# One layer change in a routed expert kernel: gathers, weight pieces, a rounding and two blocks in another order

## The chip, the core and the metric

The kernel runs on one core of a Trainium2 chip. The metric is the device time of one execution in microseconds. The core's engines are named as in the profile: PE (TensorE, matmuls), DVE (VectorE), ACT (ScalarE), POOL (GpSimd) and SP (SyncE, which here only issues DMAs). Each runs its own instructions in order and waits for the others by semaphores.

## What is computed

Three layers in a row, all in float32: a gated recurrent attention ("mixer", not touched by the change), then a mixture of experts in which each of 8 experts takes 384 of the 3072 tokens, then a two-layer ELU network over all tokens.

```python
# mixture of experts: the (token, expert) pairs in falling order of logit, each expert full at cap
cap = N // E                      # 3072 // 8 = 384
for idx in np.argsort(-(x @ w_gate).flatten()):
    tok, e = idx // E, idx % E
    if assigned[tok] < 0 and counts[e] < cap:
        assigned[tok] = e; counts[e] += 1
for e in range(E):
    h = np.maximum(x[assigned == e] @ w1[e], 0.0)      # 320 -> 1024
    out[assigned == e] = h @ w2[e]                     # 1024 -> 320
# second network, every token
h = x @ w_in                                           # 320 -> 2048
g = np.where(h > 0.0, h, np.exp(np.minimum(h, 0.0)) - 1.0)
y = g @ w_out                                          # 2048 -> 320
```

## The kernel before

The mixer fills the first 200 us or so and stores x by rows. Then the experts are done one after the other, each with its 384 tokens through both networks before the next begins. `experts_in_turn` writes the body out for experts 0 and 1, runs experts 2 to 5 in a hardware loop, two at a time, and writes out 6 and 7. The order of the work on each engine is written by hand, in one block per engine; nothing is planned by a tool.

**Two roundings.** Each float32 operand is kept as a high part, rounded by ACT, and a low part, what is left (by DVE or POOL), and a product is made of three: high by high, high by low, low by high.

**One expert on PE.** Eight hidden blocks: `up` (eight matmuls of 384 columns, a "block" of the first layer) and `down` two blocks behind. Then the change of layer, and sixteen blocks f of the second network: `up2(f)` (eight matmuls, made by `rows_product`), and `down2(f - 3)` (nine matmuls of 320 columns), three blocks behind (LAG). Three PSUM banks go round between the `up` blocks, so `up2(f)` waits for the ELU of block f - 3 (`g_ok`). In blocks 12 to 14 (TURN) PE transposes the next expert's rows (`columns`); behind the last blocks it starts the next expert's first two `up`.

**Change of layer.** `between_layers`: ACT copies a folded part (L1476), rounds two thirds of the result (L1479), then the last third (L1481, L1482); DVE adds the folded part (L1351) and makes the low parts (L1354, L1356). `up2(0)` waits part by part; its last matmul (L1622) needs L1356.

**ELU of a block.** ACT: ReLU of the negative (L1489), tanh (L1492), exp (L1497). DVE: L1362 and L1365, which gives g. ACT rounds g of the block before (`elu_hi`, L1504). POOL makes its low part (`elu_lo`, L1109). Then `down2` may start (first matmul L1684).

**Weights.** The next expert's weights come in eight pieces (0 to 3 of w1, 4 to 7 of w2), by way of two staging buffers. SP may fetch piece m when the low part of piece m - 2 is done. ACT rounds it (`piece`, L845 and L846, or L847 for w2), POOL makes the low part (`expert_rest`, L855 and L858, or L863 and L864). In the loop this happens in the even blocks 0 to 14, one piece each. For expert 0 it is done ahead of the loop: ACT rounds pieces 0 to 3, then the gathered columns, then pieces 4 to 7 with `hidden(0, 0)` behind piece 6 and `hidden(0, 1)` behind piece 7.

**Routing.** While expert k runs, DVE and PE choose expert k + 2's tokens in six rounds. Each has a comparison on DVE (the first in three slices, L756, behind the ELU of blocks 1 to 3; later ones L1194), a count on PE (L1559, or L1565 and L1573 where it is folded), a test on DVE (L1207, L1209, giving feas), the thresholds on PE (L1579), and a move of the base on DVE (L1216, L1218). During the eight hidden blocks the choice is finished: counts, ties, and the "spots" (L1320), from which PE lists the tokens (L1594) and DVE makes `idx` (L1331). POOL then gathers their rows in three indirect DMAs (L1088). The keys of the following routing (`choose_start`, `choose_keys`) stand on DVE ahead of `between_layers`. For expert 0 and 1 the rounds run ahead of the loop; `hidden(0, 0)` stands on DVE between rounds 3 and 4 of expert 1's, `hidden(0, 1)` between rounds 5 and 6.

## Time and profile before

| what | value |
|---|---|
| median of 3 runs | 884.07 us (883.91 to 884.22) |
| the profiled execution | 882.67 us, its span 880.9 us |
| PE busy | 780.1 us, 89% of the span |
| PE weight loads | 715.2 us, 81% |
| DVE busy | 547.3 us, 62% |
| ACT busy | 460.7 us, 52% |
| POOL busy | 402.7 us, 46% |
| granted TensorE clock, mean | 0.960 of full |

The rest of the 882.67 us lies around the span. The expert stage runs from about 230 us to the end. A matmul's row in the profile lasts longer than the distance to the next one, since they overlap: distances are read from start to start. A square bracket at the end of a row gives the idle time of the engine before it and what ended it.

### The profile page before, as it was taken

The page shows a single profiled execution, that of the slowest core. Times are in us where ns is not written, and L with a number is a line of the kernel's source. Part 1 is how long each engine was busy: PE and PEld are TensorE (multiplying, and loading weights), DVE is VectorE, ACT ScalarE, POOL GpSimd, SP SyncE. Part 2 cuts the span into 40 slices and gives each one's busy share as a digit, 9 for nine tenths or more (in the row PEclk, how much of TensorE's full clock was granted, in tenths as well). Part 3 has the DMA queues.
Part 4 walks back from the last instruction along what each step waited for, and adds up shares of the span by engine and source line. Part 5 has one row for each costly group of instructions (what it writes and reads, how often), then busy time and mean ns, then how long its engine had stood idle before and what let it go on. Part 6 is the DMA issues. An engine that isn't in the chain of part 4 may idle for free.

```text
span 880.9 us, 18310 instructions
## 1 busy us (share of the span) xinstructions
PE 780.1 (89%) x5822; PEld 715.2 (81%) x5822; DVE 547.3 (62%) x1586; ACT 460.7 (52%) x981; POOL 402.7 (46%) x469
## 2 busy tenths in 40 slices
PE   1999999993158999999999999999999999999994
PEld 1888888882148899889979988997898899899894
DVE  7576768686865774666577467647647664543441
ACT  1544444431231675387277538726753872784573
POOL 6544444443460464176246417624650752474133
PEclk9999999996558999999999999999999999999998
DMA  3766666633331221121122012121201212220000
GB/s 66 146 135 136 135 135 134 136 74 94 102 106 43 58 56 36 54 84 32 65 60 56 34 53 85 31 69 52 58 31 54 78 45 65 57 69 23 1 1 22
DMA packets 138516, 61.04 MB, mean 69 GB/s; under 512 B 104704, under 2 KB 136704, under 8 KB 138432
## 3 DMA queue, kind: packets, MB, share of 16 engines
q1 hardware_dynamic: 136128, 52.13, 24.5%
q0 software_dynamic: 2304, 7.87, 2.8%
q8 instruction: 43, 0.70, 0.3%
q14 instruction: 41, 0.34, 0.1%
HBM read 51.72 MB, written 8.26 MB: 68 GB/s over the span
## 4 chain that ended last, share of the span: by engine, by line
PE 45%; DVE 11%; ACT 7%; issue 5%; POOL 4%; DMA 2%; SPq 2%; ACTq 0%; DVEq 0%; POOLq 0%
PE bank L1684 6%; PE bank L1686 5%; PE bank L1685 5%; PE bank L1614 5%; PE bank L1618 5%; PE bank L1615 5%; DVE unit L1320 3%; PE bank L1622 3%; PE bank L1620 2%; DMA stage<-in_moe_w_dram 2%; PE bank L1660 2%; PE bank L1658 2%; PE bank L1659 2%; ACT unit L1492 1%; POOL xg L1088 1%
## 5 line engine op out<-in xcount | busy, mean ns | idle before, releaser
L1109 POOL TENSOR_TENSOR gl_lo<-unit,gl_hi 128x384 fp32r<-128x384 f32 x128 | 131.2, 1025 | 142.9 <-ACT gl_hi L1504 142.6
L1684 PE MATMUL bank<-Wo_hi,gl_hi 128*128 128x320 f32 x384 | 125.9, 328 | 8.2 <-POOL gl_lo L1109 8.2
L1686 PE MATMUL bank<-Wo_hi,gl_lo 128*128 128x320 f32 x384 | 118.8, 309 | 0.0
L1685 PE MATMUL bank<-Wo_lo,gl_hi 128*128 128x320 f32 x384 | 118.7, 309 | 0.0
L1362 DVE SCALAR_TENSOR_TENSOR unit<-bank,unit 128x384 f32<-128x384 f32 x104 | 57.8, 556 | 94.2 <-ACT bank L1497 86.3
L1472 ACT ACTIVATE hid_hi<-bank 128x384 fp32r<-128x384 f32 x64 | 31.4, 491 | 135.8 <-PE bank L1622 132.1
L1088 POOL DMA_INDIRECT xg<-x_rows,idx x24 | 23.3, 972 | 159.5 <-DVE idx L1331 82.9
L1614 PE MATMUL bank<-x_hi,Wi_hi 128*128 128x384 f32 x256 | 92.7, 362 | 1.9 <-DVE unit L1365 0.9
L1489 ACT ACTIVATE unit<-bank 128x384 f32<-128x384 f32 x128 | 62.0, 484 | 49.6 <-PE bank L1622 49.5
L1615 PE MATMUL bank<-x_hi,Wi_lo 128*128 128x384 f32 x256 | 86.1, 336 | 0.0
L1684 PEld LDWEIGHTS bank<-Wo_hi,gl_hi 128*128 128x128 f32 x384 | 72.6, 189 | 12.9 <-POOL gl_lo L1109 12.9
L1365 DVE TENSOR_TENSOR unit<-unit,bank 128x384 f32<-128x384 f32 x128 | 70.9, 554 | 4.4
L1685 PEld LDWEIGHTS bank<-Wo_lo,gl_hi 128*128 128x128 f32 x384 | 72.4, 188 | 0.0
L1686 PEld LDWEIGHTS bank<-Wo_hi,gl_lo 128*128 128x128 f32 x384 | 72.1, 188 | 0.0
L1492 ACT ACTIVATE unit<-unit 128x384 f32<-128x384 f32 x128 | 67.3, 525 | 4.4
L1618 PE MATMUL bank<-x_lo,Wi_hi 128*128 128x384 f32 x256 | 67.9, 343 | 1.4 <-DVE x_lo L1354 1.0
L1345 DVE SCALAR_TENSOR_TENSOR hid_lo<-bank,hid_hi 128x384 fp32r<-128x384 f32 x64 | 35.5, 554 | 53.4 <-ACT hid_hi L1472 52.8
L1504 ACT CAST gl_hi<-unit 128x384 fp32r<-128x384 f32 x128 | 63.7, 498 | 6.3 <-DVE unit L1365 6.3
L316 POOL TENSOR_SCALAR_AFFINE_SELECT W<-W 128x512 f32<-128x512 f32 x48 | 36.1, 775 | 57.7 <-ACT W L505 57.7
L444 DVE TENSOR_TENSOR PW<-bank,W 128x512 f32<-128x512 f32 x48 | 30.9, 686 | 40.5 <-PE bank L566 40.4
L1614 PEld LDWEIGHTS bank<-x_hi,Wi_hi 128*128 128x128 f32 x256 | 48.2, 188 | 8.4 <-DVE unit L1365 3.6
L1497 ACT ACTIVATE bank<-unit 128x384 f32<-128x384 f32 x104 | 51.6, 496 | 3.3
(256 smaller groups left out, 2081.8 us busy)
## 6 DMA issues: line engine op xcount, KB each, us to landing
stage<-in_moe_w_dram SPq DMA_DIRECT2D x32, 320.0 KB, 3.0
stage<-in_moe_w_dram SPq DMA_DIRECT2D x32, 256.0 KB, 2.6
stage<-in_moe_w_dram SPq DMA_DIRECT2D x96, 64.0 KB, 2.4
q_in<-in_q_dram SPq DMA_DIRECT2D x24, 160.0 KB, 2.6
k_in<-in_k_dram SPq DMA_DIRECT2D x24, 160.0 KB, 3.1
o_in<-in_o_gate_dram SPq DMA_DIRECT2D x24, 160.0 KB, 3.3
v_in<-in_v_dram SPq DMA_DIRECT2D x24, 160.0 KB, 3.4
x_rows<-xt SPq DMA_DIRECT2D x24, 160.0 KB, 1.8
```

The source lines that it names most:

```text
L1109: nc.gpsimd.tensor_tensor(gl_lo[:, b, :], ex[:, b, :], gl_hi[:, b, :].bitcast(F32), ALU.subtract).then_inc(gl_ok, 1)
L1362: nc.vector.scalar_tensor_tensor(out=ex[:, b, :], in0=exp_at(f), scalar=1.0, in1=th[:, f % 2, :], op0=ALU.add, op1=ALU.mult).then_inc(em_o ...
L1365: nc.vector.tensor_tensor(ex[:, b, :], ex[:, b, :], ring[(NF + f) % 3][:, 0:CAP], ALU.max).then_inc(g_ok, 1)
L1489: nc.scalar.activation(ex[:, b, :], ring[(NF + f) % 3][:, 0:CAP], ACT.Relu, scale=-1.0).then_inc(neg_ok, 1)
L1492: nc.scalar.activation(th[:, f % 2, :], ex[:, b, :], ACT.Tanh, scale=-0.5).then_inc(th_ok, 1)
L1504: nc.scalar.copy(gl_hi[:, b, :], ex[:, b, :]).then_inc(gl_hi_ok, 1)
L1614: nc.tensor.matmul(to, w_hi[:, c, cols], x_hi[m][:, c, :], start=(c == 0), stop=False)
L1615: nc.tensor.matmul(to, w_lo[:, c, cols], x_hi[m][:, c, :], start=False, stop=False)
L1618: nc.tensor.matmul(to, w_hi[:, c, cols], x_lo[m][:, c, :], start=False, stop=False)
L1684: nc.tensor.matmul(acc[j][:, 0:DM], gl_hi[:, f % RG, t_], Wo_hi[:, f, :], start=(f == 0), stop=False)
L1685: nc.tensor.matmul(acc[j][:, 0:DM], gl_hi[:, f % RG, t_], Wo_lo[:, f, :], start=False, stop=False)
L1686: ins = nc.tensor.matmul(acc[j][:, 0:DM], gl_lo[:, f % RG, t_], Wo_hi[:, f, :], start=False, stop=(f == NF2 - 1))
```

## The change

- The gathers of the next expert are issued on POOL after the low parts of blocks 0, 1 and 2, one each, and no longer all ahead of block 0. For expert 0 they come ahead of all its weight pieces on POOL, and ACT's columns come ahead of pieces 2 and 3.
- Pieces 0 to 6 move from the even blocks 0 to 12 to the odd blocks 3 to 15. Piece 7 (`LATE`) goes into the next expert: behind hidden block 2 on ACT, and first on POOL.
- ACT's ELU is split into `elu_tanh` and `elu_exp`; in block 1 the rounding of block 0's result stands between the two.
- `up2(0)` and `up2(1)` become `up2_first_two`: four products of block 0, four of block 1, then the low and last ones of block 0, then those of block 1.
- On DVE `choose_keys` moves behind `between_layers` and `choose_tokens`, ahead of the first ELU; the test of a folded round moves from ahead of the even block to right behind the ELU of the odd one.
- Expert 0's spots read the slots from SBUF in fp16 as all others do; the float32 copy in PSUM (`slots_p`) is gone.

The diff, without the lines that only drop the parameter `waits` of `rows_product`:

```diff
@@ -700,7 +700,6 @@
         self.cmp_w = sb("cmp", [P, G * first_n + 2], BF16)
         self.ramp1_p = bank[7][:, 176:176 + first_n]
         self.ramps_p = bank[7][:, 304:304 + (len(STEPS) - 1) * 33].rearrange("p (q n) -> p q n", n=33)
-        self.slots_p = bank[6][:, 384:512]
         self.early = sem("r_early")
         self.const, self.zeroed, self.done = sem("r_const"), sem("r_zero"), sem("r_init")
         self.first_ok = sem("r_first")
@@ -788,7 +787,6 @@
             nc.vector.tensor_scalar(self.ramps_p[:, q, 0:n], self.ramp_i[:, low:low + n],
                                     step * (1.0 if q + 1 < HIGH else UNIT), None, ALU.mult)
         nc.vector.tensor_copy(self.ramp1_p, self.ramp1[:])
-        nc.vector.tensor_copy(self.slots_p, self.slots_i[:])
         nc.vector.tensor_copy(self.slots[:], self.slots_i[:])
         nc.vector.tensor_copy(self.rows2[:], self.rows_i[:])
         nc.vector.tensor_copy(self.marks[:], self.marks_i[:])
@@ -1005,6 +1003,9 @@
     block = ctx.enter_context(nc.Block())
+    def first_expert(k):
+        return isinstance(k, int) and k == 0
+
     def passed(eng, s, value):
         if not isinstance(value, int) or value > 0:
@@ -1042,6 +1043,11 @@
     LAG = 3
     TURN = NF2 - NJ - 1
+
+    def piece_beside(f):
+        return (f - 3) // 2 if f > 2 and f % 2 else None
+
+    LATE = PER - 1
     def exp_at(f):
         return ex[:, f % RG, :] if TURN <= f < TURN + NJ else pEx
@@ -1080,13 +1086,13 @@
         for m in range(2):
             nc.gpsimd.memset(x_lo[m][W3:P, 2, :].bitcast(F32), 0.0).then_inc(x_pads, 1)
-        def gather(k, s):
-            pool.wait_ge(idx_ok, k + 1)
-            passed(pool, x_pe_part, k * NJ)
-            pool.sem_inc(pool_turn)
-            for j in range(NJ):
-                nc.gpsimd.indirect_dma_start(out=xg[:, j, :], out_offset=None, in_=x_rows[:, :],
-                                             in_offset=bass.IndirectOffsetOnAxis(ap=idx[s][:, j:j + 1], axis=0)).then_inc(x_in[j], 16)
+        def gather(k, s, j):
+            if j == 0:
+                pool.wait_ge(idx_ok, k + 1)
+                passed(pool, x_pe_part, k * NJ)
+                pool.sem_inc(pool_turn)
+            nc.gpsimd.indirect_dma_start(out=xg[:, j, :], out_offset=None, in_=x_rows[:, :],
+                                         in_offset=bass.IndirectOffsetOnAxis(ap=idx[s][:, j:j + 1], axis=0)).then_inc(x_in[j], 16)
         def scatter(k, s):
             for j in range(NJ):
@@ -1111,20 +1117,20 @@
         pool.wait_ge(x_pads, 2)
         for i in range(PI):
             rest(False, w_out_piece(i), i, i % 2, OUT_SPLIT)
+        for j in range(NJ):
+            gather(0, 0, j)
         for i in range(PER):
             expert_rest(0, i)
-            if i == 1:
-                gather(0, 0)
         def body(k, s, n, after):
-            if after:
-                pool.wait_ge(up_pe, k * UP + NF)
-                pool.wait_ge(mid_pe, k * 3 + 3)
-                gather(k + 1, 1 - s)
+            if not first_expert(k):
+                expert_rest(k, LATE)
             for f in range(NF2):
                 elu_lo(k, f)
-                if f % 2 == 0 and after:
-                    expert_rest(k + 1, f // 2)
+                if f < NJ and after:
+                    gather(k + 1, 1 - s, f)
+                if piece_beside(f) is not None and after:
+                    expert_rest(k + 1, piece_beside(f))
             scatter(k, s)
         experts_in_turn(pool, body)
@@ -1154,9 +1160,6 @@
             return (B - 1 + k) * KEY_STEPS
         SLICES = 3
-
-        def first_expert(k):
-            return isinstance(k, int) and k == 0
         def all_or_last(k):
             return (slice(G - G // B, G), G // B) if first_expert(k) else (slice(0, G), G)
@@ -1317,8 +1320,7 @@
             n = G // SPOTS
             for g in range(part * n, (part + 1) * n):
-                ins = nc.vector.tensor_scalar(spot[:, g, :], tables.slots_p if first_expert(k) else slots[:], row[:, g:g + 1],
-                                              None, ALU.is_equal)
+                ins = nc.vector.tensor_scalar(spot[:, g, :], slots[:], row[:, g:g + 1], None, ALU.is_equal)
             ins.then_inc(spot_ok, 1)
         def choose_tokens(k, s, n):
@@ -1420,24 +1422,25 @@
                 hidden(k, u)
             if after == 2:
                 choose_start(c + 1)
-                choose_keys(c + 1)
             between_layers(k)
             if after:
                 choose_tokens(c, 1 - s, n + s)
             for f in range(NF2):
                 q, odd = f // 2 - 1, f % 2
                 if after == 2:
-                    if q >= 1 and odd:
+                    if f == 0:
+                        choose_keys(c + 1)
+                    elif q >= 1 and odd:
                         if q in FOLDED:
                             round_parts(c + 1, q)
                         else:
                             round_test(c + 1, q)
                     elif q >= 2:
-                        if q - 1 in FOLDED:
-                            round_test(c + 1, q - 1)
                         round_move(c + 1, q - 1)
                         round_compare(c + 1, q)
                 elu(k, f)
+                if after == 2 and odd and q in FOLDED:
+                    round_test(c + 1, q)
                 if 1 <= f <= SLICES and after == 2:
                     compare_first(c + 1, f - 1)
                 if TURN <= f < TURN + NJ and after:
@@ -1481,7 +1484,7 @@
             nc.scalar.copy(x_hi[1][W3:2 * W3, 2, :], whole3)
             nc.scalar.copy(x_hi[1][0:W3, 2, :], whole3).then_inc(mid_hi_ok, 1)
-        def elu(k, f, after):
+        def elu_tanh(k, f):
             u, b = k * NF2 + f + 1, f % RG
             act.wait_ge(up_pe, k * UP + NF + f + 1)
@@ -1490,6 +1493,10 @@
             act.wait_ge(neg_ok, u)
             passed(act, em_ok, u - 2)
             nc.scalar.activation(th[:, f % 2, :], ex[:, b, :], ACT.Tanh, scale=-0.5).then_inc(th_ok, 1)
+
+        def elu_exp(k, f, after):
+
+            u, b = k * NF2 + f + 1, f % RG
             act.wait_ge(th_ok, u)
             passed(act, em_ok, u - 1)
             if f == TURN + NJ and after:
@@ -1510,10 +1517,12 @@
         for i in range(PI):
             piece(False, i, w_out_arrival(i), OUT_SPLIT)
-        for i in range(PE1):
+        for i in range(2):
             piece(True, i, expert_arrival(0, i), W1_SPLIT)
         for j in range(NJ):
             columns(0, j)
+        for i in range(2, PE1):
+            piece(True, i, expert_arrival(0, i), W1_SPLIT)
         for i in range(PE1):
             piece(False, i, expert_arrival(0, PE1 + i), W2_SPLIT)
             if i > 1:
@@ -1522,14 +1531,18 @@
         def body(k, s, n, after):
             for f in range(2, NF):
                 hidden(k, f)
+                if f == 2 and not first_expert(k):
+                    piece(False, LATE % PE1, expert_arrival(k, LATE), W2_SPLIT)
             between_layers(k)
             for f in range(NF2):
-                elu(k, f, after)
-                if f > 0:
+                elu_tanh(k, f)
+                if f == 1:
+                    elu_hi(k, 0)
+                elu_exp(k, f, after)
+                if f > 1:
                     elu_hi(k, f - 1)
-                if f % 2 == 0 and after:
-
-                    i = f // 2
+                i = piece_beside(f)
+                if i is not None and after:
                     piece(i < PE1, i % PE1, expert_arrival(k + 1, i), W1_SPLIT if i < PE1 else W2_SPLIT)
                 if TURN <= f < TURN + NJ and after:
                     columns(k + 1, f - TURN)
...
@@ -1665,17 +1674,35 @@
         def up2(k, f):
             r = NF + f
-            if f < 3:
-                pe.wait_ge(hid_ok, k * NF + NF - 2 + f)
+            if f == 2:
+                pe.wait_ge(hid_ok, k * NF + NF)
             else:
                 pe.wait_ge(g_ok, k * NF2 + f - 2)
-
-            def waits(c, lo):
-
+            rows_product(ring[r % 3][:, 0:CAP], Wi_hi, Wi_lo, f, 1).then_inc(up_pe, 1)
+
+        def up2_first_two(k):
+
+            to = [ring[(NF + f) % 3][:, 0:CAP] for f in range(2)]
+            for f in range(2):
+                cols = slice(f * P, (f + 1) * P)
+                pe.wait_ge(hid_ok, k * NF + NF - 2 + f)
+                for c in range(2):
+                    if f == 0:
+                        pe.wait_ge(mid_hi_ok, k * 3 + c + 1)
+                    nc.tensor.matmul(to[f], Wi_hi[:, c, cols], x_hi[1][:, c, :], start=(c == 0), stop=False)
+                    nc.tensor.matmul(to[f], Wi_lo[:, c, cols], x_hi[1][:, c, :], start=False, stop=False)
+            for f in range(2):
+                cols = slice(f * P, (f + 1) * P)
+                for c in range(2):
+                    if f == 0:
+                        pe.wait_ge(mid_ok, k * 3 + c + 1)
+                    nc.tensor.matmul(to[f], Wi_hi[:, c, cols], x_lo[1][:, c, :], start=False, stop=False)
                 if f == 0:
-                    pe.wait_ge(mid_ok if lo else mid_hi_ok, k * 3 + c + 1)
-
-            rows_product(ring[r % 3][:, 0:CAP], Wi_hi, Wi_lo, f, 1, waits).then_inc(up_pe, 1)
+                    pe.wait_ge(mid_hi_ok, k * 3 + 3)
+                nc.tensor.matmul(to[f], Wi_hi[:, 2, cols], x_hi[1][:, 2, :], start=False, stop=False)
+                if f == 0:
+                    pe.wait_ge(mid_ok, k * 3 + 3)
+                nc.tensor.matmul(to[f], Wi_hi[:, 2, cols], x_lo[1][:, 2, :], start=False, stop=True).then_inc(up_pe, 1)
         def down2(k, f):
             pe.wait_ge(gl_ok, k * NF2 + f + 1)
@@ -1728,7 +1755,9 @@
                 list_tokens(c)
             down(k, NF - 1)
             for f in range(NF2 + LAG):
-                if f < NF2:
+                if f == 0:
+                    up2_first_two(k)
+                elif 1 < f < NF2:
                     up2(k, f)
                 q = f // 2 - 1
                 routing = after == 2 and f < NF2 and q >= 1
```

## Rows read from the trace of the kernel before

**Rows 1.** Busy time by stretches, one middle expert: us, busy (x instructions), PEclk, DMA.

```profile
377.00:454.00 77.00, 74.39 (x533) 68.46 (x532) 49.65 (x154) 46.47 (x102) 36.20 (x38) 1.00 0.18 55
```

**Rows 2.** Timeline of PE at the third expert's layer change: start us, us, engine line.

```profile
443.83 0.34 PE L1660 MATMUL bank<-hid_lo,W_split 128*128 128x384 f32 x1
...
446.83 0.45 PE L1622 MATMUL bank<-x_lo,Wi_hi 128*128 128x384 f32 x1
...
450.30 0.44 PE L1614 MATMUL bank<-x_hi,Wi_hi 128*128 128x384 f32 x1 [0.24 <-DVE unit L1365]
...
453.03 0.41 PE L1684 MATMUL bank<-Wo_hi,gl_hi 128*128 128x320 f32 x1 [1.07 <-POOL gl_lo L1109]
```

**Rows 3.** Timeline, same stretch: the first block's ELU on ACT, DVE and POOL.

```profile
447.40 0.49 ACT L1489 ACTIVATE unit<-bank 128x384 f32<-128x384 f32 x1 [1.21 <-PE bank L1622]
...
448.99 0.60 ACT L845 CAST W_hi<-stage 128x512 fp32r<-128x512 f32 x1
...
449.69 0.56 DVE L1365 TENSOR_TENSOR unit<-unit,bank 128x384 f32<-128x384 f32 x1
...
451.40 0.50 ACT L1504 CAST gl_hi<-unit 128x384 fp32r<-128x384 f32 x1
...
451.98 0.99 POOL L1109 TENSOR_TENSOR gl_lo<-unit,gl_hi 128x384 fp32r<-128x384 f32 x1 [0.20 <-ACT gl_hi L1504]
```

**Rows 4.** Timeline: hand-over to the second layer, third expert, then seventh (PE).

```profile
443.13 0.48 ACT L1476 COPY unit<-bank 64x384 f32<-64x384 f32 x1 [3.29 <-PE bank L1643]
...
444.59 0.54 DVE L1351 TENSOR_TENSOR unit<-bank,unit 64x384 f32<-64x384 f32 x1
...
753.21 0.34 PE L1660 MATMUL bank<-hid_lo,W_split 128*128 128x384 f32 x1
...
755.76 0.44 PE L1622 MATMUL bank<-x_lo,Wi_hi 128*128 128x384 f32 x1
```

**Rows 5.** Timeline, third expert: two waits of PE, and DVE before the second.

```profile
468.65 0.18 PE L1579 MATMUL bank<-feas,first 128*128 128x1 bf16 x1 [0.24 <-DVE feas L1209]
...
486.55 0.55 DVE L1365 TENSOR_TENSOR unit<-unit,bank 128x384 f32<-128x384 f32 x1
...
488.14 0.18 PE L1579 MATMUL bank<-feas,first 128*128 128x1 bf16 x1 [0.49 <-DVE feas L1209]
```

**Rows 6.** Timeline, third expert: last slice of the first comparison, then its count.

```profile
457.29 1.21 DVE L756 SCALAR_TENSOR_TENSOR cmp<-hi,bank 128x1016 bf16<-128x1016 f32 x1
...
458.78 0.76 PE L1559 MATMUL bank<-pick,cmp 128*128 128x8 bf16 x24
```

**Rows 7.** The page, costliest groups: the gathers. Busy us, mean ns, idle before, releaser.

```profile
L1088 POOL DMA_INDIRECT xg<-x_rows,idx x24 | 23.3, 972 | 159.5 <-DVE idx L1331 82.9
```

**Rows 8.** Timeline of the start of the expert stage, DVE, ACT, POOL and PE.

```profile
234.05 6.29 DVE L1320 TENSOR_SCALAR unit<-bank,row 128x128 f16<-128x128 f32 x24
...
283.70 2.04 DVE L1320 TENSOR_SCALAR unit<-slots,row 128x128 f16<-128x128 f16 x12
...
235.68 0.62 ACT L845 CAST W_hi<-stage 128x512 fp32r<-128x512 f32 x1 [7.90 <-DMA stage<-in_moe_w_dram]
...
236.79 1.26 POOL L855 TENSOR_TENSOR W_lo<-stage,W_hi 128x512 fp32r<-128x512 f32 x1 [7.39 <-ACT W_hi L846]
...
242.77 1.28 POOL L1088 DMA_INDIRECT xg<-x_rows,idx  x1 [1.45 <-DVE idx L1331]
...
243.04 0.62 ACT L845 CAST W_hi<-stage 128x512 fp32r<-128x512 f32 x1 [3.74 <-DMA stage<-in_moe_w_dram]
...
246.57 1.28 POOL L855 TENSOR_TENSOR W_lo<-stage,W_hi 128x512 fp32r<-128x512 f32 x1
...
257.95 0.48 ACT L1472 ACTIVATE hid_hi<-bank 128x384 fp32r<-128x384 f32 x1
...
258.59 0.55 DVE L1345 SCALAR_TENSOR_TENSOR hid_lo<-bank,hid_hi 128x384 fp32r<-128x384 f32 x1
...
268.37 0.67 PE L1614 MATMUL bank<-x_hi,W_hi 128*128 128x384 f32 x1
```

More of the change, by code:

```diff
@@ L1607, in columns, with rows_product @@
             ins.then_inc(x_pe_part, 1)
-        def rows_product(to, w_hi, w_lo, f, m, waits):
+        def rows_product(to, w_hi, w_lo, f, m):
             cols = slice(f * P, (f + 1) * P)
             for c in range(2):
-                waits(c, 0)
                 nc.tensor.matmul(to, w_hi[:, c, cols], x_hi[m][:, c, :], start=(c == 0), stop=False)
@@ L1616, in rows_product @@
             for c in range(2):
-                waits(c, 1)
                 nc.tensor.matmul(to, w_hi[:, c, cols], x_lo[m][:, c, :], start=False, stop=False)
-            waits(2, 0)
             nc.tensor.matmul(to, w_hi[:, 2, cols], x_hi[m][:, 2, :], start=False, stop=False)
-            waits(2, 1)
             return nc.tensor.matmul(to, w_hi[:, 2, cols], x_lo[m][:, 2, :], start=False, stop=True)
```

2 lines of the change are left out of this document (1 added, 1 removed).

## Prediction

> **What bounds the kernel now.** I read the busy times by stretches first [rows 1], then PE's timeline for its holes. In a middle expert PE is busy 74.4 of 77.0 us at full granted clock, so time can be won there only where PE stands still, and in the start of the expert stage, where it hardly works. In a middle expert there are three kinds of hole.
>
> *The change of layer* [rows 2]. From the last product of the first layer (443.83) to the first output product of the second (453.03) are 9.20 us, in which PE has four blocks of eight matmuls to do, about 1.4 us each. Some 3.6 us are idle: about 1.0 before the end of block 0 (446.83), 0.4 before block 3 (450.30, waiting for DVE), 1.2 before 453.03 (waiting for POOL's low part). The last hole is ScalarE's order [rows 3]: the first ReLU starts at 447.40, DVE is through with block 0 at 450.25 (449.69 + 0.56), but gl_hi begins only at 451.40, because ACT had put a weight piece (448.99) and all three steps of block 1 ahead of it. POOL's gl_lo follows at 451.98 and PE at 453.03.
>
> *The hand-over* [rows 4]. ACT has the folded part at 443.61 (443.13 + 0.48); DVE takes it up at 444.59, behind the keys of the next routing. In the seventh expert, which makes no keys, block 0 ends 2.55 us after the last product (753.21, 755.76); in the first six it is 2.83 to 3.03 (third: 3.00).
>
> *The routing's tests* [rows 5]. PE waits 0.24 us for feas before block 8's output product and 0.49 us in block 14. The second is there in all six experts that route, 0.49 to 0.52 us.
>
> **The change part by part**, gains negative, against the profiled execution (span 880.9, 882.67 in all; the median of the three runs is 884.07, 1.4 more, and I move that by the same sum).
>
> *Keys behind the hand-over.* The eight key instructions (about 1.0 us together, by which DVE is late at 444.59 [rows 4]) move to before the first ELU, where DVE waits for ACT's exp of block 0, which ends when the piece starts (448.99) [rows 3]; that idle time hides them, and uncovered they would cost their 1.0 us per expert. Then block 0 should end 2.55 to 2.6 us after the last product, as in expert seven: -0.35 on the mean, times 6 = **-2.0**.
>
> *First two blocks interleaved.* Four products of block 1 go into the hole in front of block 0's low parts. Block 0 ends when its last x_lo comes, as before, and the ELU starts from that. PE gets 0.7 us ahead, and then waits longer before block 3, which needs DVE's result of block 0. I take it at **0** by itself; its bounds are -0.3 (the hole of 0.4 before block 3) and +0.1.
>
> *Order of ACT: ReLU and tanh of block 1, then gl_hi of block 0, then exp of block 1; weight piece in block 3 instead of 0.* Exp of block 0 ends about 449.0, where the piece starts [rows 3]. ReLU and tanh of block 1, 0.5 us each like the first ReLU, end at 450.1, before DVE is through (450.25). So gl_hi runs 450.3 to 450.8, gl_lo 450.9 to 451.9, and PE starts at 451.95 instead of 453.03: -1.1. PE is not itself later: block 3 is through at 450.30 + 1.5 = 451.8 [rows 2]. Seven experts have a piece there. The eighth has none, and gains 0.2 at most, which I leave out. What is late next is the first comparison [rows 6]: its third slice ends at 458.50 and PE counts at 458.78. The slices follow ELU 1, 2 and 3 on DVE (1.1 us each beside 1.1 us of ELU), so they move up only with exp 1, 0.3 us, and by the 0.4 that the piece took out of block 2 before: the count starts some 0.8 us earlier, not 1.1. Of the other 0.3, most comes back by block 8, where the test waits 0.24 now, since ACT has done two pieces by then and not four. So -1.1 x 7 = -7.7, with a low end of -0.8 x 7 = -5.6: I take **-7.4**.
>
> *Gathers behind the first low parts.* POOL issues the three gathers, 0.97 us each on the mean [rows 7] and 0.3 between them, now after gl_lo 0, 1 and 2, and no longer ahead of them. Queued behind each is the next gl_lo. gl_lo 0 ends at 451.9, gather 0 at 453.2, gl_lo 1 can be done at 454.4, and PE wants it after output product 0 and block 4, at 454.8: hidden by 0.4 us. The two after have over 2 us. **0**. The rows of x are wanted only in block 12.
>
> *Tests right after the odd blocks.* For q 2 to 4 DVE's order stays what it was (nothing lies between). For q = 5 it does not: the test now comes before the columns of block 13, so it can start at 487.1, when the ELU of block 13 is done [rows 5]. It takes 0.35 us, so feas is there at 487.5, when PE ends block 14 (488.14 less the wait of 0.49 and the refill of 0.1): the wait of 0.49 and the refill of 0.1 go: -0.6 x 6 = **-3.6**. Bounds -0.3 and -0.6 each.
>
> *Weight pieces later.* Pieces 0 to 6 in blocks 3 to 15, the eighth behind the next expert's hidden 2. A hidden block gives ACT one rounding of 0.5 us [rows 8] in some 2.8 us of PE (two times eight matmuls), so one piece more finds room; POOL's part stands behind the scatter, and PE wants it only with the last two of eight hidden blocks, some 17 us into the layer. **0**; without that cover 0.7 each.
>
> *The start* [rows 8] is where the change costs. The slots from SBUF in fp16 make the spots shorter: 24 took 6.29 us, and 12 of the other form took 2.04, so 24 take 4.0: idx comes 2.3 us earlier, and the first gather starts at 240.45 (was 242.77). But POOL now issues expert 0's gathers ahead of all its weight pieces, waiting for idx. Low part 0 began at 236.79; now it begins when three gathers are issued, at 240.45 + 3.80 (242.77 to 246.57) = 244.25, which is 7.5 us later. SP fetches piece 2 into its buffer only after that: from low part 0 to ACT's piece 2 were 6.25 us (236.79 to 243.04), and 1.1 more to POOL (235.68 to 236.79). So low part 2 begins at 251.6, where it was 246.57: **5.0 later**. From it a chain of two more fetches (pieces 4 and 6) leads to ACT's hidden 0, which stands behind piece 6: 11.4 us (257.95). That gives 263.0. DVE needs it (258.59 before, with no time to spare) between rounds 3 and 4 of expert 1's routing, and behind that wait stand rounds 4 to 6, whose end lets PE start block 2 (268.37). All of it moves by **+4.9**; rounds 1 to 3 finish 2.3 us earlier and wait. Bounds +4.0 and +6.0, from the spread of a fetch. PE is at the lower of its clock's two levels (1.2 and 2.4 GHz) here: that first matmul takes 0.67 us against 0.44 in row 450.30 [rows 2]. Eight of them at half the rate take about 2.8 us where 1.4 is usual, and if the rise comes one block later or earlier it is 1.4 more or less; I leave it at 0 and widen the range.
>
> By the Trainium skill, page "TensorE: Matmul & The Clock Gate", section "Part 1: The HAM clock gate", the clock follows how busy the array has been of late, in a window that runs freely; by that rule the longer stillness can't lower a clock that is low already, and the moment of the rise may shift. The 0.67 us agrees that it is low before and after; the sum is the same by rule and by row.
>
> Sum: -2.0 - 7.4 - 3.6 + 4.9 = **-8.1**; I keep 0.3 back for blocks 10 and 12, where the test is within 0.1 us of PE: -7.8. 882.67 - 7.8 = 874.9 for the profiled execution, **876.3** for the median.
>
> **The rivals.**
>
> *A start without cost.* If hidden 0 did not wait for the late pieces, 4.9 us stay in: 871.4. Against it speaks that 257.95 and 258.59 leave no slack now. 10%.
>
> *The first comparison takes the gain back.* DVE or ACT becomes the bound in blocks 3 to 8, and the 1.1 us of the routing experts are gone at the first count. Left are 2.0 + 3.6 + 1.1 (the seventh) - 4.9 = -1.8: 882.3. For it: PE's count follows the last slice by 0.3 us already [rows 6]. Against it: exp 1 comes earlier too. 15%, half of it inside 0.2%.
>
> *The gathers hold the low parts up: slower.* Each gather stands between two low parts. If it holds POOL for g us longer than its 0.97, beside DVE's ELU and comparison, gl_lo 3 is late by 3g - 2.5 in all seven experts (its slack is 2.5 us). The gain is gone at g = 1.2, and with g = 1.6 (a gather of 2.5 us) it is 7 x 2.3 = 16 us: 892. Against it: the mean of all 24 is 0.97 us [rows 7], and DVE works beside most of them now. For it: the very first one [rows 8] took 1.28. 8%.
>
> By the skill's page "SBUF — State Buffer", section "Who interferes with whom", writing a gather's descriptors is shut out while VectorE runs a two-port instruction, and that would be this rival; it also says that an instruction with a PSUM operand does not do it, which is what stands beside the gathers here, and no row of before shows a gather so held.
>
> The change as I read it, 876.3: 67%.
>
> **How the numbers follow.** A measurement of this kernel can tell 0.2%, 1.8 us: 882.3 to 885.8 is "the same". Faster: 67% + 10% + half of 15% = 84%, less 2% for what I haven't seen: 0.82. Same: 0.09. Slower: 0.09. The range goes from the start without cost (871.5) to the lost comparison (882.0). It leaves out the slower case and the tips of the other two.
>
> **What would show it.** Right: gl_hi of block 0 directly behind tanh of block 1, PE's first output product 4.9 to 5.1 us after block 0's last matmul (it was 6.0 to 6.2); block 0's end 2.6 us after the last product; no wait of L1579 in block 14; hidden 0 of expert 0 at 263 and block 2 at 273. Wrong: a PE wait of 1 us before the first count of each expert, gathers over 2 us, a hidden 0 that stays at 258, or a new PE hole in blocks 3 to 8.

## The result and the profile after

| | before | after |
|---|---|---|
| median | 883.99 us (882.93 to 884.22, 4 runs) | 873.54 us (872.99 to 874.11, 4 runs) |
| profiled execution, its span | 882.67, 880.9 | 872.99, 871.2 |
| PE's first count of expert 0 | 208.71 | 207.43 |
| *start*: from there to the last product of expert 0's first layer | 81.56 | 87.93 |
| *behind*: from there to the end of the span | 590.63 | 575.84 |

The ratio is 0.9884, interval [0.9867, 0.9901]: 10.4 us faster. 876.3 was forecast, with 871.5 to 882.0 around it. The three lower rows divide the span, and all runs below are read by them. The mixer, which nothing here touches, ends at different times from profile to profile (first count between 207.43 and 211.73), so a difference of 1 or 2 us in one median may be its doing; *start* and *behind* are free of it. Of the 9.7 us between the spans, -1.3 is the mixer, +6.4 the start and -14.8 what lies behind. For the last two the forecast was +4.9 and -12.7.

Timeline of PE of the kernel after, the third expert's layer change and its test in block 14 (start us, us, line, [idle before <- what ended it]); it answers [rows 2, 5, 6]:

```profile
444.67 0.34 PE L1669 MATMUL bank<-hid_lo,W_split 128*128 128x384 f32 x1
...
447.25 0.42 PE L1705 MATMUL bank<-x_lo,Wi_hi 128*128 128x384 f32 x1
...
450.68 0.45 PE L1626 MATMUL bank<-x_hi,Wi_hi 128*128 128x384 f32 x1 [0.92 <-DVE unit L1367]
...
452.31 0.41 PE L1711 MATMUL bank<-Wo_hi,gl_hi 128*128 128x320 f32 x1
...
486.67 0.18 PE L1592 MATMUL bank<-feas,first 128*128 128x1 bf16 x1
```

From the last product to block 0's last matmul are 2.58 us (3.00 before), and 7.64 to the first output product (9.20). The wait for POOL's low part is gone from the row 452.31; the wait for DVE ahead of block 3 (row 450.68) has grown from 0.24 to 0.92, and it is now the largest hole of the change of layer. The row of the test in block 14 has no bracket: PE waits no more. ACT, DVE and POOL, same stretch, answering [rows 3]:

```profile
449.88 0.52 ACT L1495 ACTIVATE unit<-unit 128x384 f32<-128x384 f32 x1
450.66 0.51 ACT L1511 CAST gl_hi<-unit 128x384 fp32r<-128x384 f32 x1 [0.25 <-DVE unit L1367]
451.08 0.49 ACT L1504 ACTIVATE bank<-unit 128x384 f32<-128x384 f32 x1
...
450.07 0.56 DVE L1367 TENSOR_TENSOR unit<-unit,bank 128x384 f32<-128x384 f32 x1
...
451.25 1.01 POOL L1115 TENSOR_TENSOR gl_lo<-unit,gl_hi 128x384 fp32r<-128x384 f32 x1 [20.73 <-ACT gl_hi L1511]
452.41 0.98 POOL L1094 DMA_INDIRECT xg<-x_rows,idx  x1 [0.15 <-issue]
453.57 1.02 POOL L1115 TENSOR_TENSOR gl_lo<-unit,gl_hi 128x384 fp32r<-128x384 f32 x1 [0.17 <-ACT gl_hi L1511]
```

gl_hi runs as soon as DVE is through with block 0 and not 1.2 us later, gl_lo behind it, and the gather (0.98 us) fits between two low parts: the second low part waits for ACT (0.17), not for the gather. The start, answering [rows 8]:

```profile
232.60 3.99 DVE L1323 TENSOR_SCALAR unit<-slots,row 128x128 f16<-128x128 f16 x24
...
239.01 1.29 POOL L1094 DMA_INDIRECT xg<-x_rows,idx  x1 [11.06 <-DVE idx L1333]
...
242.81 1.28 POOL L853 TENSOR_TENSOR W_lo<-stage,W_hi 128x512 fp32r<-128x512 f32 x1
...
249.95 0.62 ACT L843 CAST W_hi<-stage 128x512 fp32r<-128x512 f32 x1 [3.36 <-DMA stage<-in_moe_w_dram]
...
251.05 1.26 POOL L853 TENSOR_TENSOR W_lo<-stage,W_hi 128x512 fp32r<-128x512 f32 x1 [4.38 <-ACT W_hi L844]
...
262.34 0.48 ACT L1475 ACTIVATE hid_hi<-bank 128x384 fp32r<-128x384 f32 x1
...
265.25 0.34 PE L1578 MATMUL bank<-pick,cmp 128*128 128x32 bf16 x6 [7.76 <-DVE cmp L1197]
...
272.53 0.67 PE L1626 MATMUL bank<-x_hi,W_hi 128*128 128x384 f32 x1
```

POOL stands idle for 11.06 us, issues the gathers, and only then makes the first low part. Hidden 0 comes last, and behind it the routing: PE waits 7.76 us in one hole.

### The profile page after: what moved, and what is told of

The parts are those of the page before. It is cut to its first block, busy times and chain, and to the rows that moved or that the text cites. A ratio compares the mean times of both kernels' runs of the same rounds, so it can differ in the third digit from the quotient of the medians.

```text
span 871.2 us, 18302 instructions
## 1 busy us (share of the span) xinstructions
PE 773.0 (89%) x5822; PEld 716.4 (82%) x5822; DVE 546.6 (63%) x1585; ACT 461.9 (53%) x981; POOL 403.7 (46%) x469
## 4 chain that ended last, share of the span: by engine, by line
PE 60%; DVE 9%; ACT 2%; issue 2%; POOL 1%; DMA 1%; SPq 0%; ACTq 0%; DVEq 0%; POOLq 0%
PE bank L1711 7%; PE bank L1626 7%; PE bank L1629 6%; PE bank L1627 6%; PE bank L1713 6%; PE bank L1712 6%; PE bank L1631 3%; PE bank L1630 3%; PE bank L1667 3%; PE bank L1669 3%; PE bank L1668 3%; DVE cmp L755 3%; DVE unit L1364 2%; PE bank L1652 1%; PE bank L1655 1%
## 5 line engine op out<-in xcount | busy, mean ns | idle before, releaser
L1364 DVE SCALAR_TENSOR_TENSOR unit<-bank,unit 128x384 f32<-128x384 f32 x104 | 57.8, 556 | 84.0 <-ACT bank L1504 84.0
L1626 PE MATMUL bank<-x_hi,Wi_hi 128*128 128x384 f32 x224 | 80.4, 359 | 6.7 <-DVE unit L1367 6.7
L1627 PE MATMUL bank<-x_hi,Wi_lo 128*128 128x384 f32 x224 | 75.2, 336 | 0.0
L316 POOL TENSOR_SCALAR_AFFINE_SELECT W<-W 128x512 f32<-128x512 f32 x48 | 36.1, 776 | 56.8 <-ACT W L505 56.8
L1629 PE MATMUL bank<-x_lo,Wi_hi 128*128 128x384 f32 x224 | 57.3, 337 | 0.0
L491 ACT COPY xT<-bank 128x384 f32<-128x384 f32 x24 | 11.5, 478 | 76.7 <-PE bank L610 76.7
L1626 PEld LDWEIGHTS bank<-x_hi,Wi_hi 128*128 128x128 f32 x224 | 42.2, 188 | 9.2 <-DVE unit L1367 9.2
```

The source lines that it names most:

```text
L1364: nc.vector.scalar_tensor_tensor(out=ex[:, b, :], in0=exp_at(f), scalar=1.0, in1=th[:, f % 2, :], op0=ALU.add, op1=ALU.mult).then_inc(em_o ...
L1626: nc.tensor.matmul(to, w_hi[:, c, cols], x_hi[m][:, c, :], start=(c == 0), stop=False)
L1627: nc.tensor.matmul(to, w_lo[:, c, cols], x_hi[m][:, c, :], start=False, stop=False)
L1629: nc.tensor.matmul(to, w_hi[:, c, cols], x_lo[m][:, c, :], start=False, stop=False)
```

## The experiments

All medians stand against runs of the kernel before on the same chip (883.67 to 884.57). *Start* and *behind* come from each profiled execution.

| kernel | median, us | ratio, 95% | start | behind |
|---|---|---|---|---|
| before | 883.99 | | 81.56 | 590.63 |
| after | 873.54 | 0.9884 [0.9867, 0.9901] | 87.93 | 575.84 |
| e1_hidden_early | 868.04 | 0.9820 [0.9803, 0.9837] | 80.44 | 576.04 |
| u3_gathers_first | 878.49 | 0.9945 [0.9925, 0.9966] | 86.87 | 580.26 |
| u1_hi_behind_exp | 872.99 | 0.9878 [0.9857, 0.9899] | 87.65 | 574.76 |
| u2_pieces_even | 893.21 | 1.0114 [1.0092, 1.0136] | 87.24 | 595.84 |
| u7_pieces_and_gathers | 883.56 | 0.9982 [0.9965, 0.9999] | 86.72 | 584.15 |
| u4_keys_before | 876.76 | 0.9929 [0.9906, 0.9953] | 86.88 | 577.82 |
| u5_tests_even | 882.02 | 0.9974 [0.9959, 0.9990] | 86.74 | 582.74 |
| u6_blocks_apart | 874.59 | 0.9899 [0.9875, 0.9923] | 85.61 | 575.78 |
| e2_gather_behind_two | 873.31 | 0.9881 [0.9855, 0.9906] | 86.81 | 576.13 |
| b1_early_and_hi_behind | 865.47 | 0.9793 [0.9772, 0.9813] | 79.21 | 574.86 |
| b2_early_hi_two | 866.85 | 0.9815 [0.9789, 0.9841] | 81.33 | 574.81 |
| b3_early_hi_slots_psum | 867.38 | 0.9815 [0.9790, 0.9840] | 81.39 | 574.52 |

The start as the change made it shows the scatter of such a reading: eight kernels have it (after, and the u kernels), from 85.61 to 87.93, 86.96 on the mean. The kernel after is the longest of them, and of the start before there is one reading. *Behind* scatters by about 0.3 (575.78 to 576.13 in four kernels that differ in nothing that matters there). The u kernels each undo one part of the change and keep the rest.

**The cost of the start.** e1 puts hidden 0 of expert 0 ahead of ACT's second four pieces; all else stays.

```diff
+        hidden(0, 0)
                 ...
-            if i > 1:
-                hidden(0, i - 2)
+            if i == 0:
+                hidden(0, 1)
```

> The changed kernel with one thing moved on ACT, ahead of the loop: hidden 0 of expert 0 stands behind weight piece 3 (no longer behind piece 6) and hidden 1 behind piece 4. Theory of the forecast (DVE's rounds 4 to 6 wait for hidden 0, which waits for the late weight pieces): the 7.8 us that PE stands still between rounds 3 and 4 go to about 0, the first block of expert 0 behind round 6 starts at 264.3 instead of 272.5, and the kernel takes 865.2 us (8.3 less than 873.5). Rival (the late pieces themselves are what PE needs): the wait reappears before the first products with w2 and the gain is under 4 us, 870 or more.

The start fell to 80.44, 6.5 below the mean of 86.96, and the hole of 7.76 us is gone: the row of that count (260.22) has no bracket.

```profile
256.49 0.47 ACT L1475 ACTIVATE hid_hi<-bank 128x384 fp32r<-128x384 f32 x1
...
260.22 0.39 PE L1579 MATMUL bank<-pick,cmp 128*128 128x32 bf16 x6
...
267.54 0.67 PE L1627 MATMUL bank<-x_hi,W_hi 128*128 128x384 f32 x1
```

The mechanism holds, but the size came out smaller: 868.04 where I had 865.2, a gain of 5.5 us by the medians and not 8.3. I had taken the hole from the kernel after; in the eight kernels with this start it is 6.5 to 7.9 us. So the start waits for hidden 0, and hidden 0 for the pieces ahead of it on ACT. What makes these late is a question of its own. e2 keeps hidden 0 behind piece 6 and puts POOL's gathers back behind the low parts of pieces 0 and 1:

```diff
-        for j in range(NJ):
-            gather(0, 0, j)
         for i in range(PER):
             expert_rest(0, i)
+            if i == 1:
+                for j in range(NJ):
+                    gather(0, 0, j)
```

> The changed kernel with one part undone, in the start alone: POOL issues expert 0's three gathers behind the low parts of weight pieces 0 and 1, as the kernel before did, and not ahead of all of them. Hidden 0 keeps its new place behind piece 6 on ACT. Measured from PE's first count of expert 0 to the last product of its first layer, the start takes 81.6 us before and 87.0 on the mean of the eight kernels with the new start. My theory (the chain gathers, low part 0, fetch of piece 2, low part 2, pieces 4 and 6, hidden 0): low part 0 goes back to about 236, hidden 0 of expert 0 to about 257, and the start to 80.9 to 81.9; the rest of the kernel stays 575.8; ratio 0.982. Rival (the cost lies in ACT's new order, columns ahead of pieces 2 and 3, or in POOL's three gathers wherever they stand): the start stays over 85 and the ratio at 0.988.

My theory failed here: 86.81, where I had 80.9 to 81.9. DVE, POOL and ACT of this kernel:

```profile
234.43 6.62 DVE L1324 TENSOR_SCALAR unit<-slots,row 128x128 f16<-128x128 f16 x24
...
243.47 1.28 POOL L1094 DMA_INDIRECT xg<-x_rows,idx  x1 [1.78 <-DVE idx L1334]
...
247.70 0.37 ACT L1465 CAST x_hi<-bank 128x256 fp32r<-128x256 f32 x1 [8.04 <-PE bank L1620]
...
250.96 0.62 ACT L843 CAST W_hi<-stage 128x512 fp32r<-128x512 f32 x1
...
262.95 0.48 ACT L1476 ACTIVATE hid_hi<-bank 128x384 fp32r<-128x384 f32 x1
```

The low parts of pieces 0 and 1 do come early again, and piece 2 is fetched in time: its row on ACT (250.96) has no wait for a DMA. But ACT now takes the gathered columns ahead of piece 2, stands 8.04 us idle for them, and comes to piece 2 at 250.96, 41.3 us behind the first count. It was 42.5 in the kernel after, where POOL made it late, and 34.3 before. The change has two reasons for a late hidden 0: POOL's gathers ahead of the low parts, and ACT's columns ahead of pieces 2 and 3. I had priced the first and not the second. In the kernel after ACT is through with the columns and ready for piece 2 at 246.59 (249.95 less its wait of 3.36), which is 39.2 us behind the first count: the columns alone make piece 2 4.8 us later than before, and POOL's late low part adds 3.4. In e2 the columns alone made it 7.0, because there the gathers too come 2.2 us later than in the kernel after (33.8 us behind the first count, not 31.6), for the reason that follows. No run has POOL's new order with ACT's old one, so that POOL's part by itself is argued from its wait of 3.36 us.

The row of the spots holds a second surprise: 6.62 us, not 3.99. b2 shows it again. Below is the spots' tile in b2, then the form with slots in PSUM in the kernel before (duration ns min/median/max, first and last start us):

```profile
L1324 DVE TENSOR_SCALAR unit<-slots,row x24: 242/249/1308, 232.5 to 237.9; 128x128 f16<-128x128 f16 x24
```

```profile
L1320 DVE TENSOR_SCALAR unit<-bank,row x24: 343/343/351, 234.1 to 240.0; 128x128 f16<-128x128 f32 x24
```

In b2 POOL makes low parts beside the spots, of two instructions each (1.26 and 0.72 us, from 235.30 and from 237.84). Twenty-one of the 24 spots take 0.24 to 0.25 us. The other three start within 0.03 us of an instruction of POOL and end within 0.06 us of its end: 1.31 us from 235.31, 0.76 from 236.53 and 1.28 from 237.87. In e2 it is again three spots (1.28, 0.76 and 1.32 us). So a spot that meets a low part of POOL is held for the length of that instruction. Before, the same low parts (from 236.79 and 239.38) ran beside the PSUM form, and none of the 24 took over 351 ns.

The Trainium skill's page "SBUF — State Buffer", section "Who interferes with whom", says that a `tensor_scalar` in a two-port mode and a GpSimd instruction exclude each other for the whole instruction. The trace agrees, with 1308 ns for one spot, though no row tells the mode.

So the slots in SBUF are worth 2.3 us only because the gathers stand ahead of the low parts and POOL is idle beside the spots; with both low parts beside them they cost 0.3 (6.61 against 6.29).

**Gathers and pieces in the loop.** u3 issues all three gathers ahead of the first low part, u2 puts the pieces back into the even blocks 0 to 14, u7 does both. u3:

```diff
+            if after:
                 ...
+                for j in range(NJ):
+                    gather(k + 1, 1 - s, j)
             for f in range(NF2):
                 elu_lo(k, f)
-                if f < NJ and after:
-                    gather(k + 1, 1 - s, f)
```

> The changed kernel with the three gathers of the loop put back ahead of low part 0, all else as changed. The forecast gave this move 0 us: 873.5. Rival (POOL was a second lock of nearly the same height: in the kernel before the gathers ended at 451.8 and gl_hi at 451.9, so freeing ACT alone frees nothing): the first output product comes 1.1 us later in seven experts, 7.50 to 7.65 us after the last product of layer one become 8.6 to 8.8, and the kernel takes 873.5 + 7 x 1.1 = 881 us, less what the first count's wait of 0.27 us takes up in six of them: 879.5 to 881.

u2 (in u7 with the lines of u3):

```diff
-        return (f - 3) // 2 if f > 2 and f % 2 else None
+        return None if f % 2 else f // 2
-            if not first_expert(k):
-                expert_rest(k, LATE)
                 ...
```

> The changed kernel with the weight pieces back in the even blocks 0 to 14, none in the next expert. Theory of the forecast: the piece in block 0 puts ReLU and tanh of block 1 and gl_hi of block 0 0.9 us later in seven experts; the test before block 8 is late again by some 0.3. 873.5 + 7 x 0.9 + 6 x 0.2 = 881. Rival (the gathers alone made the 1.1 us): 873.5 to 875.

> The changed kernel with both put back: weight pieces in the even blocks 0 to 14 and the three gathers ahead of low part 0. Each alone cost: the pieces 19.3 us, the gathers 3.4 us (expert stage, counted from PE's first count to the end, 663.8 us in the changed kernel and 672.2 before). Theory 1 (the two stand in for each other: a gather between low parts is bearable only where no weight piece stands there too, on POOL): the stage is near that of the kernel before, less the earlier keys and tests, plus the longer start: 671 to 673 us, 11 less than with the pieces alone. Theory 2 (the costs add up): 686 us. Theory 3 (the even blocks as such cost the 19 us, by ACT): 683 us.

Behind the start, u3 costs 4.4, u2 20.0 and u7 8.3. For u3 the rival's mechanism came true and not its price: the first output product comes at 8.59 us (8.6 to 8.8 expected), but the first count only 0.5 us later, and 4.4 are lost instead of 6 to 7.5. For u2 my 881 was wrong by 12 us (893.21); I had priced only ACT's queue. For u7 theory 1 holds: from the first count to the end are 670.9 us, where it had 671 to 673, and not 683 or 686. In u3 the third gather still holds POOL when gl_hi is ready; POOL and PE:

```profile
451.45 0.95 POOL L1094 DMA_INDIRECT xg<-x_rows,idx  x1 [0.30 <-issue]
452.42 1.00 POOL L1115 TENSOR_TENSOR gl_lo<-unit,gl_hi 128x384 fp32r<-128x384 f32 x1
...
453.48 0.41 PE L1714 MATMUL bank<-Wo_hi,gl_hi 128*128 128x320 f32 x1 [0.92 <-POOL gl_lo L1115]
```

Most of what ACT's order wins at the first output product would be lost again at POOL (8.59 for 7.64, 0.95 us). Before, the gathers stood there without harm, since gl_hi was itself late [rows 3]. In u2 POOL has a gather and a piece's low part between the first two gl_lo:

```profile
457.66 1.01 POOL L1115 TENSOR_TENSOR gl_lo<-unit,gl_hi 128x384 fp32r<-128x384 f32 x1 [23.05 <-ACT gl_hi L1509]
458.81 0.99 POOL L1094 DMA_INDIRECT xg<-x_rows,idx  x1
459.82 1.30 POOL L853 TENSOR_TENSOR W_lo<-stage,W_hi 128x512 fp32r<-128x512 f32 x1
461.08 0.74 POOL L856 TENSOR_TENSOR W_hi<-stage,W_hi 128x256 fp32r<-128x256 f32 x1
461.77 0.99 POOL L1115 TENSOR_TENSOR gl_lo<-unit,gl_hi 128x384 fp32r<-128x384 f32 x1
...
462.82 0.42 PE L1707 MATMUL bank<-Wo_hi,gl_hi 128*128 128x320 f32 x1 [1.12 <-POOL gl_lo L1115]
...
468.02 0.62 ACT L843 CAST W_hi<-stage 128x512 fp32r<-128x512 f32 x1 [3.16 <-DMA stage<-in_moe_w_dram]
```

The second gl_lo starts 4.1 us after the first (2.3 after the change), and PE waits. The low part of piece 0 ends 0.8 us later than in u7 (11.29 us after the last product for 10.48), and so is the fetch of piece 2 later: ACT stands 3.16 us for it in block 4, with the ELU queued behind. Over the seven experts this wait is 1.8 to 3.2 us, in u7 0.6 to 2.1. The third expert is 1.5 us behind the kernel after at its first count (15.11 for 13.61) and 3.1 at the test of block 8 (26.21 for 23.14), and loses no more behind that. How the 3.1 divide between PE's waits for gl_lo and ACT's for the fetch is not shown: the experts are 2.7 to 3.0 us longer whether ACT stands 1.8 us or 3.2.

u2 is slower than before by 1.1%, the only kernel here that is. Counted from u7, where neither move is made, the pieces' move alone (u3) wins 3.9 us, the gathers' move alone (u2) loses 11.7, and both together win 8.3. The two moves have to be priced as one.

**The other parts.** u1 puts the rounding of block 0 behind both steps of block 1:

```diff
-                if f == 1:
-                    elu_hi(k, 0)
-                if f > 1:
+                if f > 0:
```

> The changed kernel with gl_hi of block 0 back behind exp of block 1. Theory of the forecast: ACT is 0.3 us later with gl_hi in all eight experts, the first output product too; in the six experts that route exp 1 and with it the three slices of the first comparison come 0.5 us earlier, so the count's wait of 0.27 us pays for it. Net +0.1 us each there and +0.3 in the last two: +1 us, 874.5. Rival (the order within block 1 is what gained the 1.1 us, not the piece and the gathers): +7 us, 880.

*Behind* fell by 1.1, where I had expected 1 more (the medians, 872.99 and 873.54, are too close to tell; b1, b2 and b3, which have the same order, show 574.5 to 574.9 too). In the third expert the first output product is 0.2 later (7.85 instead of 7.64), but the first count is 0.24 earlier (13.37 instead of 13.61), and the time from expert to expert goes with the count: 0.26 less in the experts that route, 0.2 more in the last two. ACT's exp of block 1, ahead of the rounding, starts DVE's ELU 1 sooner, and the first comparison's slices stand behind that. u4 moves the keys back to where they were:

```diff
+                choose_keys(c + 1)
                 ...
-                    if f == 0:
-                        choose_keys(c + 1)
                 ...
```

> The changed kernel with the keys back ahead of the hand-over on DVE. Forecast: block 0 ends 0.35 us later (2.9 behind the last product of layer one instead of 2.58) in the six experts that route, all else shifts with it: expert stage 663.8 + 2.1 = 665.9 us. Rival (the first count, which waits 0.27 us for DVE's third slice, takes the gain up; the slices follow the same chain): under +0.5.

2.0 us *behind*, as forecast. u5 puts the tests of the folded rounds back ahead of the even block:

```diff
+                        if q - 1 in FOLDED:
+                            round_test(c + 1, q - 1)
                 ...
-                if after == 2 and odd and q in FOLDED:
-                    round_test(c + 1, q)
```

> The changed kernel with the folded rounds' tests back at the start of the even blocks. Forecast: PE waits for feas in block 14 again, 0.6 us in six experts: expert stage 663.8 + 3.6 = 667.4 us, all of the difference between the thresholds of blocks 12 and 14. Rival (the pieces' new places alone free ACT and DVE by then): +0 to +0.5.

It cost 6.9 *behind*, nearly twice the 3.6: per expert 1.1 us at block 14, and nothing up to block 12. ACT, DVE and PE of u5:

```profile
487.24 0.73 ACT L845 CAST W_split<-stage 128x640 fp32r<-128x640 f32 x1
...
488.51 0.26 ACT L1466 CAST x_hi<-bank 64x128 fp32r<-64x128 f32 x1
...
488.81 0.42 DVE L1339 TENSOR_TENSOR x_lo<-bank,x_hi 128x256 fp32r<-128x256 f32 x1 [0.69 <-ACT x_hi L1466]
489.15 0.27 DVE L1341 TENSOR_TENSOR x_lo<-bank,x_hi 64x128 fp32r<-64x128 f32 x1
489.34 0.14 DVE L1210 TENSOR_TENSOR over<-bank,rem 31x8 f32<-31x8 f32 x1
...
489.73 0.18 PE L1592 MATMUL bank<-feas,first 128*128 128x1 bf16 x1 [0.97 <-DVE feas L1212]
```

ACT's piece stands now in block 13, ahead of the columns. DVE waits 0.69 us for these, and in u5 the test is queued behind them: PE waits 0.97 us where it was 0.49 [rows 5]. So the test's move also wins back what the pieces' move would have lost. u6 makes the first two blocks one after the other:

```diff
-            to = [ring[(NF + f) % 3][:, 0:CAP] for f in range(2)]
+                to = ring[(NF + f) % 3][:, 0:CAP]
                 ...
-            for f in range(2):
-                cols = slice(f * P, (f + 1) * P)
```

> The changed kernel with blocks 0 and 1 of the second network one after the other again. Forecast (the interleave is worth 0, since block 3 waits for block 0's ELU in any case): the wait before block 3 falls from 0.92 to 0.2 us and nothing else moves: expert stage 663.8 us, within 0.3. Rival (block 1's ReLU is now reached earlier by ACT, so a block 1 that ends 0.7 us later delays ACT, gl_hi 0 and the first output product): +0.2 to +0.5 per expert, 665.5 to 668.

*Behind* is 575.78 against 575.84, and the wait before block 3 falls from 0.92 to 0.24 us (0.2 expected): the interleave is worth nothing, as forecast.

**A better kernel.** b1 joins e1 and u1; b2 puts the gathers of expert 0 behind two low parts in it, as in e2; b3 puts its slots back into PSUM:

```diff
-                ins = nc.vector.tensor_scalar(spot[:, g, :], slots[:], row[:, g:g + 1], None, ALU.is_equal)
+                ins = nc.vector.tensor_scalar(spot[:, g, :], tables.slots_p if first_expert(k) else slots[:], row[:, g:g + 1], None, ALU.is_equal)
                 ...
```

> A kernel meant to beat both: the changed kernel with expert 0's hidden 0 ahead of ACT's pieces 4 and 6 (as in the run that took the cost of the start away, whose start was 80.4 us), and with ACT's rounding of block 0 behind both steps of block 1 (as in the run that took 1.1 us off the part behind). If the two add: start 80.4, the part from the last product of expert 0's first layer to the end 574.8 (changed kernel 575.8), the time 866.5 to 868.5 with the mixer's own scatter of 1 to 2 us, ratio 0.980 to 0.982. If the rounding's place is worth nothing and its 1.1 us were scatter: that part stays at 575.6 to 576.2.

> The last kernel with one part more: expert 0's gathers behind the low parts of pieces 0 and 1. Hidden 0 no longer waits for late pieces there, so the place of the gathers should matter little: if hidden 0 is bound by the gathers' arrival and the columns, it comes up to 1 us later (the start 80.4 to 81.5). If the pieces were still what it waits for, the start would get shorter, 78 to 80. The part behind stays as in the last one.

> The kernel two above (hidden 0 early, rounding behind both steps), but expert 0's spots read the slots from PSUM in float32 again, as before the change. My term was 2.3 us for 24 spots (6.29 against 4.0). With hidden 0 bound by the gathers, the whole 2.3 us should show in the start: 82.7 instead of 80.4. If something else binds the start (the rounds of the routing on DVE, PE's counts), less than 1 us shows. The part behind stays.

b1 is the fastest: 865.47 us, 8 below the kernel after and 2.1% below the kernel before. *Behind* is 574.86 (574.8 expected), the start 79.21 (80.4 expected). In b3 the start is 2.2 longer than in b1 (2.3 expected), though at 81.39 it is not the 82.7 that I had: with hidden 0 out of the way, the start is bound by the routing behind the spots. DVE takes hidden 0 up in b1 without a wait. In b2 the start is 2.1 longer; its 81.33 lies in my 80.4 to 81.5, but for another reason: hidden 0 comes 0.9 earlier than in b1 (45.4 us behind the first count, not 46.3), and what counts is that the spots beside POOL's low parts take 6.61 us again. The same start code gave 80.44 in e1 and 79.21 in b1, so 2 us in one reading of the start is not much; the shorter stretch from the first count to block 2's first matmul says it more clearly: 57.4 and 56.8 us in e1 and b1, 59.3 and 59.1 in b2 and b3. By the medians the three kernels lie within their scatter of each other (864.6 to 868.1); it is the parts that tell them apart.

## Why the prediction was right, point by point

- *Keys*: right. -2.0 was forecast, undoing it cost 2.0, and block 0 ends 2.58 us after the last product, where I had 2.55 to 2.6.
- *ACT's order*: the chain came out as written. I had gl_hi at 6.5 us after the last product, POOL at 7.1, PE at 8.1, less the 0.4 of the keys; it was 5.99, 6.58 and 7.64. The term was -7.4, and undoing pieces and gathers together costs 8.3 (u7). Where I put the first count 0.8 earlier by this term, it is 1.3 earlier with the keys' 0.4 in it (13.61 for 14.95), 0.9 by itself. I left out that the order inside block 1 is itself a trade: the rounding ahead of exp delays ELU 1 and with it the first comparison, and u1 shows that this costs 1.1 us more than it wins.
- *Gathers at nothing*: right in the kernel as changed (0.98 us each, the next low part waiting for ACT, 0.17). But the 0 is only half of it. Had they stayed where they were, 4.4 of ACT's gain would have been lost (u3), and I did not say that the two go together.
- *Tests*: the size was right, -0.6 per expert: from block 8's to block 14's test are 18.86 us, 19.49 before. It is the tests' own doing, since u7, with the pieces and gathers where they were, has 18.82 there. What I hadn't seen is that the piece now in block 13 makes the old place of the test dearer, 1.1 by u5.
- *The parts together*: u7 is the kernel before with keys, tests, interleave and the order inside block 1 alone, and its *behind* is 6.5 us less (584.15 for 590.63), where the forecast had 2.0 + 3.6 = 5.6. The pieces and gathers then bring the 8.3 that were forecast as 7.4. With the 0.3 that I kept back these two are the 2.1 us by which I was too low. Undone one by one, keys (2.0), tests (6.9), pieces with gathers (8.3) and the order inside block 1 (-1.1) give 16.1, not the 14.8 that they bring together. Part of u5's 6.9 comes up only beside the piece in block 13 (0.5 per expert); how the rest overlaps no run separates.
- *The interleave*: 0, and 0 by u6. Its price is visible and harmless: the wait ahead of block 3.
- *Pieces later at nothing*: right; no wait for them shows in the experts' periods.
- *The start*: +4.9 was forecast, and it was +5.4 by the mean of 86.96, against one reading before. Up to block 2's first matmul it is +4.6 on the mean of the eight (64.3 us behind the first count for 59.7); the other 0.8 lie behind it, where PE's clock rose up to some 3 us later than before and which I had left at 0. In the profile of the kernel after, against the first count, idx is 2.5 us earlier (2.3 forecast), the first low part 7.3 later (7.5), low part 2 5.8 later (5.0), hidden 0 5.7 later (5.0). The excess is the fetch of piece 2: 7.14 us from low part 0 to ACT's piece, where [rows 8] had 6.25. That is scatter and no error of the term: u1 has 7.2 too, and the six other kernels with this start have 6.2 to 6.4. But the step had a hole that its number hid: ACT's columns ahead of piece 2 take 4.8 of the 8.2 us by which ACT is late there, so that the mechanism I named was not the only one.
- *A reading*: I named three holes of 1.0, 0.4 and 1.2 us in the change of layer, which is less than the 3.6 of idle time that I stated. The 3.00 us to the end of block 0 hold 1.6 and not 1.0, with eight products of 0.175 us to do. No term of the sum used it.
- *The rivals*: a start without cost fell by the 7.76 us hole. The first comparison did not take the gain back; the count is 1.2 to 1.3 us earlier in each routing expert. The gathers did not hold the low parts up. The gain behind the start was forecast 2.1 us too small and the cost of the start 0.5 to 1.5 too small, so the two errors partly cancel in the total, and the mixer gave 1.3 by chance. That the time lies no further than 2.8 us from the forecast is in part luck.

## What to carry to other kernels

Price a group of moves on in-order queues as a group: the gathers' new place won 4.4 us with the pieces moved, and lost 11.7 with the pieces where they had been (595.84 against 584.15); what differs is what else stood in POOL's and ACT's queues. When a long chain ends in one wait, walk it back on every engine before naming the cause, since taking one cause away may leave another of the same length. And ask of an instruction with both operands in SBUF what POOL does beside it before trusting its duration.

## What the runs showed of the hardware that I had not expected

- A spot of 0.25 us is held for up to 1.31 us by a POOL instruction of 1.26 us beside it, while the same work with its input in PSUM, 0.34 us, is not held at all. An ELU step of DVE with both inputs in SBUF is held too: in u5 L1364 of block 14 takes 1.20 us in each of six experts, where 0.56 is its usual time, beside a gl_lo of POOL of 1.00 us. It begins behind the test, and PE does not wait for it.
- The granted clock rose at a moment that does not follow the hole. From block 2's first matmul PE's rows stay at the lower of the two levels (1.2 and 2.4 GHz) for 2.7 us before (from 268.37), some 4.7 us after, with its hole of 7.76 us, but also 5 us in e1, which has no such hole, and 2.7 us in u6, which has one of 6.59. From there to the last product of the first layer it was 21.9 to 23.4 us over all fourteen kernels, and over the eight with the same start as well. The 0.9 us that the kernel after has over before in that stretch lie within the scatter of the rise; I can't lay them to the change.
- The mixer's end moved by up to 4.3 us between the profiles of kernels that run the same mixer. Executions of one and the same kernel lie up to 4.9 us apart as well (u5, 878.69 to 883.58), so this need not be a difference of the kernels. The cause stays open.
